# Start addresses of the large on-chip tiles: from 256 or 288 bytes behind a multiple of 512 to 128 bytes

## The reference

```python
# 1. attention in chunks of 32 queries: 16 keys left, 8 right, 8 memory keys; 4 x 8 heads of 64
scores = scale * q_c @ k_full.T
a = exp(scores - max) ; a = a / (sum(a) + 1e-9)
x = a @ v_full                         # 3072 x 512
# 2. one dense layer pair with a rational activation
h = x @ w_in                           # 512 -> 2048
g = (a0 + a1*h + a2*h*h + a3*h*h*h) / (1 + |b0|*|h| + |b1|*h*h + 1e-6)
x = g @ w_out                          # 2048 -> 512
# 3. eight experts, each token goes to the one with the largest gate logit
expert = argmax(x @ w_gate) ; gate_w = softmax(x @ w_gate)[expert]
out = gate_w * (relu(x @ w1[expert]) @ w2[expert])   # 512 -> 1024 -> 512
```

## Time and profile before

| | us |
|---|---|
| median of 3 runs (1079.6 to 1080.15) | 1079.87 |
| the profiled execution | 1079.0 |
| its span, from the first to the last instruction | 1077.3 |
| TensorE busy within the span | 1015.9 |

### The profile page before, as it was taken

How to read it: one execution, slowest core, us unless ns; L and a number is a source line. 1 busy time by engine, 2 the same in 40 slices (tenths; PEclk the granted TensorE clock), 3 DMA queues, 4 the chain that set the end, 5 groups by cost and what they waited for, 6 DMA issues and landing times.

```text
span 1077.3 us, 20008 instructions
## 1 busy us (share of the span) xinstructions
PE 1015.9 (94%) x6221; PEld 818.0 (76%) x6222; DVE 650.2 (60%) x1207; ACT 583.0 (54%) x1255; POOL 407.5 (38%) x397
## 2 busy tenths in 40 slices
PE   8988999999999999999999999349999999999995
PEld 5766778888888888888888887338888888888884
DVE  6877788768767876886787677705234255222221
ACT  7877778766666666676667666314133145212210
POOL 3775454444534453554455345501111111111111
PEclk9999999999999999999999999769999999999998
DMA  8999410001100110110010032165115150111110
GB/s 307 358 414 337 183 40 21 20 1 40 40 0 10 39 29 0 39 39 0 10 39 10 1 118 78 60 211 219 49 39 185 49 195 30 39 43 39 39 49 24
DMA packets 33311, 92.71 MB, mean 86 GB/s; under 512 B 4327, under 2 KB 10087, under 8 KB 33264
## 3 DMA queue, kind: packets, MB, share of 16 engines
q1 hardware_dynamic: 26464, 70.54, 18.1%
q0 software_dynamic: 6800, 21.56, 5.9%
HBM read 71.08 MB, written 21.79 MB: 86 GB/s over the span
## 4 chain that ended last, share of the span: by engine, by line
PE 87%; DVE 4%; ACT 4%; issue 2%; DMA 1%; SPq 1%; POOL 0%; POOLq 0%; ACTq 0%; DVEq 0%
PE PS L463 25%; PE PS L562 24%; PE PS L652 15%; PE PS L686 14%; ACT prob L727 2%; PE PS L672 2%; PE PS L582 2%; PE PS L515 1%; PE PS L637 1%; DVE PS L894 1%; DMA qk<-qk_all 1%; PE PS L594 1%; PE PS L485 1%; ACT out_t L718 1%; SPq L334 0%
## 5 line engine op out<-in xcount | busy, mean ns | idle before, releaser
L463 PE MATMUL PS<-xs,weights 128*128 (+1 forms) x1152 | 287.4, 398 | 0.0
L463 PEld LDWEIGHTS PS<-xs,weights 128*128 128x128 f32 x1152 | 213.0, 188 | 47.3
L562 PE MATMUL PS<-weights,g_hi 128*128 128x512 f32 x768 | 241.7, 396 | 3.4 <-POOL g_lo L1196 3.4
L1196 POOL TENSOR_TENSOR g_lo<-g_sb,g_hi 128x512 fp32r<-128x512 f32 x96 | 124.1, 1293 | 291.0 <-ACT g_hi L776 291.0
L562 PEld LDWEIGHTS PS<-weights,g_hi 128*128 128x128 f32 x768 | 143.4, 188 | 41.2 <-POOL g_lo L1196 5.6
L562 PE MATMUL PS<-weights,g_lo 128*128 128x512 f32 x384 | 151.6, 395 | 0.0
L757 ACT ACTIVATE b_ln<-PS,cf 128x512 f32<-128x512 f32 x96 | 66.0, 688 | 157.8 <-PE PS L463 157.7
L652 PE MATMUL PS<-weights,xg_hi 128*128 x448 | 144.8, 405 | 2.6 <-DVE xg_lo L1118 2.6
L686 PE MATMUL PS<-weights,h_hi 128*128 x432 | 138.2, 401 | 0.3 <-issue 0.3
L1199 POOL TENSOR_TENSOR den<-den,b_r 128x512 f32<-128x512 f32 x96 | 124.1, 1292 | 2.1 <-ACT b_r L784 2.1
L1118 DVE TENSOR_TENSOR xg_lo<-PS,xg_hi 128x512 fp32r<-128x512 f32 x29 | 20.0, 690 | 153.2 <-ACT xg_hi L801 153.2
(11 more groups left out here) (184 smaller groups left out, 1583.3 us busy)
## 6 DMA issues: line engine op xcount, KB each, us to landing
e_raw<-w_exp SPq DMA_DIRECT2D x35, 512.0 KB, 6.3
qk<-qk_all SPq DMA_DIRECT2D x32, 480.0 KB, 6.6
vw<-v_all SPq DMA_DIRECT2D x32, 384.0 KB, 6.1
w_raw<-w_mlp SPq DMA_DIRECT2D x16, 512.0 KB, 7.5
xg<-rows_by_expert POOLq DMA_DIRECT2D x30, 257.0 KB, 3.0
x_raw<-attention_out_t SPq DMA_DIRECT2D x10, 512.0 KB, 4.1
attention_out_t<-out_t SPq DMA_DIRECT2D x12, 384.0 KB, 5.8
x_raw<-w_exp SPq DMA_DIRECT2D x5, 512.0 KB, 3.3
```

What stands on the lines that cost most here:

```text
L463: last = pe.matmul(PS[:, H_BANK + f % 2, :], w[:, wp], rhs, start=k == 0, stop=k == 3 * KT - 1)
L562: last = pe.matmul(PS[:, ACC_BANK + s, :], gp[:, f % 2, s * P:(s + 1) * P], w[:, wp], start=f == 0 and k == 0, stop=f == FT - 1 and k == 2)
L1196: pool.tensor_tensor(g_lo[:, q], g_sb[:], g_hi[:, q].bitcast(F32), ALU.subtract).then_inc(g_lo_done, 1)
```

## The change

Five places are edited, and all of them move addresses only:

```diff
+PAD_RAW, PAD_X2 = 96, 120
+XG = 640
...
+        sb("before_x", [P, PAD_RAW])
         x_raw = sb("x_raw", [P, KT, TB // 2])
...
             x2 = sb("x2", [P, SUBS, XW], F32, ph)
+            sb("beside_x2", [P, PAD_X2], F32, ph)
+            x2_t = sb("x2_t", [P, KT, P], F32, ph)
             place = sb("place", [P, SUBS], U32, ph)
-            x2_t = sb("x2_t", [P, KT, P], F32, ph)
...
-            sb("xg_kept", [P, XW], F32, ph)
+            sb("xg_kept", [P, XG], F32, ph)
...
-            xg = sb("xg", [P, XW], F32, ph)
+            xg = sb("xg", [P, XG], F32, ph)
...
-                pool.dma_start(xg[:], tiles_dram[bass.ds(col, 1)].rearrange("o p n -> (o p) n")).then_inc(gathered, 16)
+                pool.dma_start(xg[:, 0:XW], tiles_dram[bass.ds(col, 1)].rearrange("o p n -> (o p) n")).then_inc(gathered, 16)
```

## The result

The changed kernel takes 1064.69 us (median of 4 runs, 1063.91 to 1065.39), the kernel before 1079.73 in the same comparison. The ratio is 0.9862, its 95% interval 0.9845 to 0.9879: 15 us or 1.4% faster, where I had forecast no change, in a range that ended at 1077.0. Lines of the changed kernel stand four further down than before (L467 is L463 of before, L566 is L562, L656 is L652, L690 is L686).

What follows compares the result with a forecast made beforehand. TensorE's pace of 233.3 ns over 3624 matmuls was taken to bound the kernel, 845 of 1077.3 us. All terms summed to 0, so no change from the median, 1079.9 us, at 75%; eight-in-ten range 1077.0 to 1082.6 us.

Steps and rivals of the forecast that it cites:

- What bounds the kernel: Whole kernel: 3624 matmuls at 233.3 ns make 845 of 1077.3 us; only their pace, or stage 1 and the gap, could matter.
- The streaming and the stationary operand by themselves: 512-column matmuls of stages 2 and 3: moving either operand's start address to remainder 128 costs 0 ns.
- Both at the same remainder: 512-column matmuls whose two operands share a remainder: taken as 0, from 48 equal pairs in L502's transposes at 272 to 273 ns.
- The unexplained 20 ns: 512-column matmuls: pace of 233 ns stands 20 ns above the 213 ns derived from 384-column, 16-bit matmuls.
- rival B: Matmuls of stages 2 and 3: pace above column rate comes from addresses and goes, 72 us less, 1007 us; chance 3%.
- B's second objection: Against the address explanation of the 20 ns: the series giving 213 ns for 512 columns is of 16-bit numbers.
- Rival A: Matmuls of stages 2 and 3: equal remainders make TensorE's two reads collide, 4 ns each, 14 us slower, 1094 us; chance 5%.
- Stationary operands, bounds of 1.5 us either way: Stationary operands moved to 128: value 0, at most 0.4 ns each way, 1.5 us over 3624 matmuls.
- VectorE, ScalarE, GpSimd: Copies and splits, such as those of `e_raw`: new addresses cost 0, bound +0.8 us; L1014 (L1010 before) keeps 1218 ns.
- DMAs: Loads and stores beginning 128 bytes behind a multiple of 256: cost 0, windows showing under 1%; skill's rule estimated 0.3 us.
- Stage 1: Start of the kernel, where engines wait in a ring: re-timed order, value 0, bounds -2.0 and +1.0 us.
- re-timing: Stage 1 or the gap falls into another rhythm: 3.5 us less, 1076.4 us, chance 9%; opposite 3.3 us more, 5%.

Runs made afterwards that it cites:

- experiment 1: Own kernel, TensorE alone, series of 24 matmuls over all 32-byte remainders of both operands: equal by 256 bytes about 5.45 us, most others 5.59 us.
- experiment 2: Changed kernel with 128 more bytes ahead of the weights, so every large tile begins 256 behind a multiple of 512: 1062.91 us, ratio 0.9844.
- experiment 10: Changed kernel with 384 more bytes ahead of the weights, so all large tiles begin at multiples of 512: 1063.56 us, ratio 0.9846.
- experiment 5: Own kernel, TensorE alone, varying fine offsets, alternating remainders, streaming widths and 16-bit numbers: 226.7 to 234 ns a matmul over 20 offsets, 16-bit 216 ns.
- experiment 11: Own kernel, TensorE alone, series of 48 with alternating remainders and 128 to 32 stationary columns: equal pairs 227.7 ns at 128 columns, 230.0 at 96.
- experiment 8: Changed kernel itself measured once more, all large tiles at 128, beside the versions at 256 and at 0: 1064.11 us, ratio 0.9854.
- experiment 9: Changed kernel with all large tiles moved to 256, measured once more in the same comparison as those at 128 and 0: 1064.17 us, ratio 0.9850.
- experiment 6: Changed kernel with 128 bytes more behind xs, so g_hi, g_lo and the tiles behind them in stages 1 and 2 return to 256: 1071.30 us, ratio 0.9911.

## Why the prediction was wrong

**What bounds the kernel:** right. The two things that could move the time were named, and 14.3 of 14.9 us came from the first, the pace of the 3624 matmuls.

**The streaming and the stationary operand by themselves:** right as far as they went. Experiments 1, 2 and 10 show that no place is good or bad in itself.

**"Both at the same remainder", taken as 0:** this step failed. I had noted that no 512-column matmul of before had an equal pair, and then let a 128-column row stand for it, the 48 equal pairs of L502. Experiment 5 shows why it could not: with 256 streaming columns the address costs nothing measurable, and L502 streams 128. Experiment 11 adds the other half, since the stationary operand of L502 has 96 columns: there equal remainders take 230.0 ns and not 226.7. The term's value was -3.9 ns a matmul over all 3624 (14.3 us by 3624), -6.6 in undisturbed series. I had read an untested state as a tested one: 233.3 ns for differences of 128 and 160 was two samples of unequal pairs, not proof of a floor.

**The unexplained 20 ns:** rival B held the right clue, 233 against a column rate of 213, and was dismissed with 3% because "the excess is the same for pairs 128 and 160 bytes apart". That is the same mistake once more. Its price was off too: 6.6 of the 20 ns went, not all. The other 13 stay at every remainder tried. B's second objection, that the 213 come from 16-bit numbers, holds in part: at this very shape 16-bit numbers take 216 ns in experiment 5, 11 ns less than the best 32-bit pair. Rival A had the mechanism the wrong way round: equal remainders do not collide, they are the ones that don't cost.

**Stationary operands, bounds of 1.5 us either way:** too narrow for the same reason; they were drawn from rows that all had unequal pairs.

**VectorE, ScalarE, GpSimd:** right. L1014 keeps 1216 ns, and one chunk still takes 1450 beside GpSimd, now as then. The splits of `e_raw` on ScalarE and GpSimd take 1043 and 2340 ns, before 1044 and 2348. **DMAs:** right, by the windows above and by experiments 8 to 10. The rule of the Trainium skill, "DMA: Bandwidth & Descriptors", section "How a descriptor splits into AXI transactions", that the bytes ahead of an unaligned start still cost would by my estimate have made the kernel with everything at 128 slower by 0.3 us than the one at 256; no run here can tell 0.3 us, and the medians are 0.06 apart. **Stage 1:** its ends moved by 0.4 us, within the bounds.

**The range** reached 2.9 us down from the forecast, because I gave 9 of the 12% on the faster side to re-timing. With B's own number, 72 us, the honest price for an untested operand pair was anything from 0 to 72 us.

## What to carry to other kernels

Where a kernel runs at TensorE's pace with 32-bit operands, 128x128 stationary and 512 columns streaming, lay both operands' tiles at the same remainder by 256 bytes: a few padding tiles gave 1.4% here. At 384 streaming columns 2 ns were left of the gain, with 64 stationary columns nothing. Check it by the pace in the chain, 12 matmuls in 2.72 us against 2.80, and if the pace stands above the column rate for no visible reason, vary the addresses before calling it a floor. A row at another shape is no evidence for the shape that matters: a short series of TensorE alone, with the very shape and type, costs one run and shows which addresses are fast. How much of that arrives in the kernel, 15 of 24 us here, the kernel itself must show.

## What was not expected of the hardware

- The pace of 32-bit 128x128 by 512 matmuls depends on the difference of the operands' start addresses, with a period of 256 bytes: 226.7 ns at 0, 229.6 where the stationary start is 192 above the streaming one, 233 to 234 at the other multiples of 32. By smaller steps it is irregular (252: 226.7, 248: 233.3, 240: 228.8).
- 16-bit numbers at the same shape run at 216 ns at difference 0 and 128 alike.
- Behind other matmuls, a matching series often needs seven to nine matmuls before it reaches its pace: 24 in stage 3 take 5.49 us, not 5.44, and in experiment 6, behind an unequal series, 12 take 2.76, not 2.72. It is not always so: `stay_i` in experiment 1 runs at 227 ns from its first matmul, though the series before it is unequal.
- With 96 or 64 stationary columns the matching pair runs at 230 ns, slower than with 128 columns, though the load is shorter (161 and 134 ns against 188).
